# Second-layer chunks of 512 tokens in place of 256, with the second layer's tiles laid over those of attention and the first layer

## The chip, the cores and the metric

The kernel runs on one core of one Trainium2 chip. The time is that of the device for one execution of the program, in microseconds (us). Three runs of the kernel before gave 686.68, 687.62 and 688.28 us; their median, 687.62 us, is what the changed kernel is compared with.

## What is computed

Attention with a sliding window and four sink keys, over 2 sequences of 768 tokens with 8 heads of 64, gives x of 1536 tokens by 512 features. Two feed-forward layers follow, each 512 -> 2048 -> 512. In the second, the hidden values pass through an exponential linear unit. The reference, cut to what matters here:

```python
def _attn_ref(q, k, v, n_sink, window):
    scores = scale * np.matmul(q, k.transpose(0, 1, 3, 2))
    keep = is_sink | in_window
    ...
    return np.matmul(a, v).astype(np.float32)

def _moe_ref(x, w_in, w_out):
    h = x @ w_in
    g = np.where(pos, h, np.where(neg, 0.0, (h + beta) ** 2 / (4.0 * beta)))
    return (g @ w_out).astype(np.float32)

def _moe2_ref(x, w_in, w_out):
    h = x @ w_in
    g = np.where(h > 0.0, h, alpha * (np.exp(np.minimum(h, 0.0)) - 1.0))
    return (g @ w_out).astype(np.float32)
```

## The kernel before

**Tiling.** Tokens lie along the free dimension and features on the partitions. The 1536 tokens are cut into NC = 6 chunks of CT = 256. A product of a layer is made three times over, since every fp32 operand is split into a high and a low part of type fp32r: high x high, high x low, low x high. TensorE holds a 128x128 block of weights and streams one chunk of tokens past it.

**A layer on a chunk.** `layer_chunk` goes over FT = 16 blocks t of the hidden features. `hidden(t)` makes h_t with 12 matmuls (lines 445 to 447: 4 blocks of input features, 3 products each) in one of two PSUM banks `h_ps`. `outward(t)` adds block t to y with 12 matmuls (lines 458 to 460: 4 blocks m of output features, 3 products each). On TensorE the order is hidden(t), outward(t - 2), hidden(t + 1), outward(t - 1) and so on, and a chunk ends with outward(13), outward(14), outward(15). `hidden(t)` waits until VectorE has finished with the bank of h_(t-2) (semaphore `g_ready`); `outward(t)` waits for the low part of g_t (`g_lo_ready`).

**The activation of the second layer.** ScalarE takes relu(-h) into `ramp` (line 589) and exp of its negative into `g_full` (line 591); VectorE makes g = max(e - 1, h) (line 748); ScalarE rounds it to `g_hi` (line 579); VectorE takes the rest, `g_lo` (line 733). g_hi and g_lo are rings of GR = 3 tiles.

**Between chunks.** ScalarE and VectorE split the next chunk's x into `x_hi` (line 573) and `x_lo` (line 728), four blocks k each. ScalarE then waits for the end of outward(15) and copies y out of its two banks, 2 x 512 columns (`write_y`, line 597), since a bank holds two blocks m of 256 tokens. The copies for the last chunk are followed by the last two stores of SyncE's queue (line 336).

**Order of the stages.** Attention of chunk 0 comes first. Attention of chunk c + 1 is then spread over the first layer's chunk c. The last chunk of the first layer has no attention beside it; there the second layer's weights replace the first's, one 128x1024 piece at a time (`split_weights`, lines 563 and 722), and three pieces are left for the second layer's first chunk. Each piece comes by a 512 KB load into one of RAW = 6 raw buffers: two of their own and four lent by tiles of attention. The second layer is the loop `pe.Fori(NC, 2 * NC)` over six chunks.

Every order on an engine is the order in which the code is written; engines meet only at semaphores.

Of the kernel before, what the change touches and what calls it, by code (L numbers as in the profile page):

```python
# [23 lines left out]
F32 = mybir.dt.float32  # L24
# [5 lines left out]
P = 128  # L30
# [5 lines left out]
CPB = SEQ // CT  # L36
QB = CT // P
# [42 lines left out]
def build(nc, q_t, k_t, v_w, v_s, w_in, w_out, ident_d, out, n_sink, window):  # L80
# [8 lines left out]
    with ExitStack() as ctx:  # L89
# [26 lines left out]
        probs_t = sb("probs_t", [P, 2, 512])
        sinks_t, vsink_parts = sb("sinks_t", [P, CT], F32R), sb("vsink_parts", [P, P], F32R)
        masks, mask = sb("masks", [P, 2, QB * MW], BF16), sb("mask", [P, QB * MW], BF16)
# [4 lines left out]
        half = small[:, 4 * QB:4 * QB + 1]  # L123

# [13 lines left out]
        h_ready, y_step = sem("h_ready"), sem("y_step")  # L138
# [11 lines left out]
        def chunk(c):  # L150
            return xy[:, :, bass.ts(c, CT)]
# [40 lines left out]
        def pairs_before(c, p):  # L192
# [14 lines left out]
        place = [i if i < FEW else (i - FEW) % RAW for i in range(NW)] + [i % RAW for i in range(NW)]  # L207
# [49 lines left out]
        def _(sp):  # L257
# [125 lines left out]
        def _(pe):  # L383
# [50 lines left out]
            def hidden(layer, c, t):  # L434
# [5 lines left out]
                o = h_ps[t % 2][:, 0:CT]  # L440
# [9 lines left out]
            def outward(layer, c, t):  # L450


                pe.wait_ge(w_lo_ready, at[layer * NW + 2 * (t // 2) + 1] + 1)
                pe.wait_ge(g_lo_ready, c * FT + (t + 1))
                for m in range(KT):
                    o = y_ps[m // 2][:, (m % 2) * CT:(m % 2 + 1) * CT]
                    cols = slice(m * P, (m + 1) * P)
                    pe.matmul(o, wout_hi[:, t, cols], g_hi[:, t % GR, :], start=(t == 0 and m % 2 == 0), stop=False, skip_group_check=True)  # L458
# [33 lines left out]
            with pe.Fori(NC, 2 * NC) as c:  # L492
                layer_chunk(1, c)
# [3 lines left out]
        def _(act):  # L497
# [67 lines left out]
            def split_x(layer, c, at_chunk, features=range(KT)):  # L565

                for k in features:
                    if layer == 0:
                        act.wait_ge(x_written, c * PAIRS + (k + 1))
                    else:  # L570
                        act.wait_ge(y_written, (at_chunk + 1) * len(y_ps))
# [277 lines left out]
```

## Time and profile before

| what | value |
|---|---|
| median of three runs | 687.62 us (686.68 to 688.28) |
| span of the profiled execution, first to last instruction | 685.2 us |
| its own time, by the span and the about 2.4 us that the median has beyond it | about 687.6 us |
| TensorE matmuls busy | 662.4 us, 97% |
| TensorE weight loads busy | 648.7 us, 95% |
| VectorE busy | 407.8 us, 60% |
| ScalarE busy | 388.3 us, 57% |
| mean granted TensorE clock | 1.000 |

The profile is of one execution. A matmul's recorded duration is modelled and overlaps the next one's, so the pace of TensorE is read from the distance between two starts. PEld is the weight load that goes ahead of each matmul. Busy time is a sum over the whole span; the second layer is the stretch from 403.17 us on.

### The profile page before, as it was taken

Reading aid. Unit: us, or ns where it says so; the run is one execution under the profiler, and the core shown is the slowest. Engines: PE = TensorE matmul, PEld = TensorE weight load, DVE = VectorE, ACT = ScalarE, POOL = GpSimd, SP = SyncE. Lnnn points to the kernel's source line nnn. Section 1 sums busy time; section 2 is a strip of 40 time slices with the busy share of each in tenths; the row PEclk is TensorE's granted clock in tenths of the full one; section 3 lists DMA queues with packets and bytes.
Section 4 is the critical chain, followed back from the end, with each engine's and each line's share of the span. In section 5 each row is a group of like instructions: output and inputs, shape, how many; then the busy total and the mean of one; then the engine's idle time right before and its main releaser. Section 6 shows DMA issues by size and latency. Waiting matters only on the chain.

```text
span 685.2 us, 15326 instructions
## 1 busy us (share of the span) xinstructions
PE 662.4 (97%) x5356; PEld 648.7 (95%) x5356; DVE 407.8 (60%) x1130; ACT 388.3 (57%) x1010; POOL 9.7 (1%) x28
## 2 busy tenths in 40 slices
PE   4889999999999999999999999999999999999997
PEld 3679899999999999999999999999999999999997
DVE  6989976885887588678847864232332322323321
ACT  6877855665656566566655665454454544544443
POOL 3000000000000000000000000000000000000000
PEclk9999999999999999999999999999999999999999
DMA  8468222231332032223125500000000000000000
GB/s 275 170 221 293 67 67 61 76 90 41 89 92 83 23 108 67 65 66 89 43 111 173 182 28 1 2 31 0 0 31 0 31 0 0 31 0 0 31 0 31
DMA packets 27339, 47.39 MB, mean 69 GB/s; under 512 B 2928, under 2 KB 14000, under 8 KB 27312
## 3 DMA queue, kind: packets, MB, share of 16 engines
q1 hardware_dynamic: 27312, 47.03, 22.0%
q8 instruction: 16, 0.26, 0.2%
q14 instruction: 11, 0.09, 0.0%
HBM read 43.88 MB, written 3.15 MB: 69 GB/s over the span
## 4 chain that ended last, share of the span: by engine, by line
PE 87%; DVE 10%; issue 1%; ACT 1%; DMA 0%; ACTq 0%; SPq 0%; DVEq 0%
PE h_ps L445 13%; PE y_ps L458 13%; PE h_ps L447 13%; PE h_ps L446 13%; PE y_ps L460 13%; PE y_ps L459 13%; PE o_ps L424 2%; PE t_ps L403 2%; PE s_ps L391 1%; PE s_ps L392 1%; DVE wout_lo L722 1%; PE o_ps L426 1%; PE o_ps L425 1%; DVE s_ps L676 1%; DVE win_lo L722 1%
## 5 line engine op out<-in xcount | busy, mean ns | idle before, releaser
L445 PE MATMUL h_ps<-x_hi,win_hi 128*128 128x256 f32 x768 | 220.4, 287 | 1.1 <-DVE x_lo L728 0.5
L458 PE MATMUL y_ps<-g_hi,wout_hi 128*128 128x256 f32 x768 | 218.2, 284 | 1.1 <-DVE g_lo L733 1.1
L460 PE MATMUL y_ps<-g_hi,wout_lo 128*128 128x256 f32 x768 | 217.3, 283 | 0.0
L459 PE MATMUL y_ps<-g_lo,wout_hi 128*128 128x256 f32 x768 | 217.3, 283 | 0.0
L447 PE MATMUL h_ps<-x_hi,win_lo 128*128 128x256 f32 x768 | 216.9, 282 | 0.0
L446 PE MATMUL h_ps<-x_lo,win_hi 128*128 128x256 f32 x768 | 216.8, 282 | 0.0
L445 PEld LDWEIGHTS h_ps<-x_hi,win_hi 128*128 128x128 f32 x768 | 146.5, 191 | 3.7 <-DVE g_full L744 1.0
L458 PEld LDWEIGHTS y_ps<-g_hi,wout_hi 128*128 128x128 f32 x768 | 147.3, 192 | 2.7 <-DVE g_lo L733 1.3
L459 PEld LDWEIGHTS y_ps<-g_lo,wout_hi 128*128 128x128 f32 x768 | 147.4, 192 | 0.0
L460 PEld LDWEIGHTS y_ps<-g_hi,wout_lo 128*128 128x128 f32 x768 | 147.3, 192 | 0.0
L446 PEld LDWEIGHTS h_ps<-x_lo,win_hi 128*128 128x128 f32 x768 | 146.8, 191 | 0.0
L447 PEld LDWEIGHTS h_ps<-x_hi,win_lo 128*128 128x128 f32 x768 | 146.7, 191 | 0.0
L748 DVE SCALAR_TENSOR_TENSOR g_full<-g_full,h_ps 128x256 f32<-128x256 f32 x96 | 40.4, 421 | 138.4 <-ACT g_full L591 138.4
L579 ACT CAST g_hi<-g_full 128x256 fp32r<-128x256 f32 x192 | 77.7, 405 | 78.2 <-DVE g_full L748 46.1
L733 DVE TENSOR_TENSOR g_lo<-g_full,g_hi 128x256 fp32r<-128x256 f32 x192 | 81.3, 424 | 67.4 <-ACT g_hi L579 66.7
L589 ACT ACTIVATE ramp<-h_ps 128x256 f32<-128x256 f32 x96 | 36.7, 382 | 88.8 <-PE h_ps L447 88.8
L516 ACT ACTIVATE probs<-s_ps,small 128x260 f32<-128x260 f32 x84 | 39.2, 470 | 22.7 <-DVE small L679 22.6
L586 ACT ACTIVATE ramp<-h_ps,small 128x256 f32<-128x256 f32 x96 | 45.5, 474 | 7.0 <-PE h_ps L447 6.8
L742 DVE SCALAR_TENSOR_TENSOR g_full<-ramp 128x256 f32<-128x256 f32 x96 | 40.4, 420 | 10.2 <-ACT ramp L586 9.8
L744 DVE TENSOR_TENSOR g_full<-g_full,h_ps 128x256 f32<-128x256 f32 x96 | 40.4, 421 | 3.3
L591 ACT ACTIVATE g_full<-ramp 128x256 f32<-128x256 f32 x96 | 40.1, 418 | 3.1
L522 ACT COPY probs_t<-t_ps 128x512 f32<-128x512 f32 x42 | 24.7, 587 | 28.1 <-PE t_ps L403 27.9
(126 smaller groups left out, 704.7 us busy)
## 6 DMA issues: line engine op xcount, KB each, us to landing
ks<-in_k SPq DMA_DIRECT2D x44, 260.0 KB, 2.7
vs<-in_v SPq DMA_DIRECT2D x24, 288.0 KB
qs<-in_q SPq DMA_DIRECT2D x44, 128.0 KB, 2.5
raw<-in_w_in SPq DMA_DIRECT2D x6, 512.0 KB, 4.0
raw<-in_w_out SPq DMA_DIRECT2D x6, 512.0 KB, 4.1
out_y<-xy SPq DMA_DIRECT2D x12, 256.0 KB, 2.3
xy<-in_w_in SPq DMA_DIRECT2D x5, 512.0 KB, 6.3
xy<-in_w_out SPq DMA_DIRECT2D x5, 512.0 KB, 6.7
```

What stands on the lines that cost most here:

```text
L445: pe.matmul(o, win_hi[:, k, f], x_hi[:, k, :], start=(k == 0), stop=False)
L446: pe.matmul(o, win_hi[:, k, f], x_lo[:, k, :], start=False, stop=False)
L447: last = pe.matmul(o, win_lo[:, k, f], x_hi[:, k, :], start=False, stop=(k == KT - 1))
L458: pe.matmul(o, wout_hi[:, t, cols], g_hi[:, t % GR, :], start=(t == 0 and m % 2 == 0), stop=False, skip_group_check=True)
L459: pe.matmul(o, wout_hi[:, t, cols], g_lo[:, t % GR, :], start=False, stop=False, skip_group_check=True)
L460: last = pe.matmul(o, wout_lo[:, t, cols], g_hi[:, t % GR, :], start=False, stop=(t == FT - 1), skip_group_check=True)
L579: nc.scalar.copy(g_hi[:, t % GR, :], g_full[:, t % 2, :]).then_inc(g_hi_ready, 1)
L586: nc.scalar.activation(ramp[:, t % 2, :], h, ACT.Relu, bias=half[:, 0:1], scale=0.5).then_inc(ramp_ready, 1)
L733: nc.vector.tensor_tensor(g_lo[:, t % GR, :], g_full[:, t % 2, :], g_hi[:, t % GR, :].bitcast(F32), ALU.subtract).then_inc(g_lo_ready, 1)
L742: nc.vector.scalar_tensor_tensor(g, r, 1.0, r, ALU.min, ALU.mult).then_inc(bent_ready, 1)
L744: nc.vector.tensor_tensor(g, g, h, ALU.max).then_inc(g_ready, 1)
L748: nc.vector.scalar_tensor_tensor(g, g, -1.0, h, ALU.add, ALU.max).then_inc(g_ready, 1)
```

## The change

The second layer takes chunks of CT1 = 512 tokens, NC1 = 3 of them. Its matmuls stream 512 columns, and its activation, splits and copies are 512 wide. Its tiles (`g1_hi`, `g1_lo`, `ramp1`, `g1_full`, `x1_hi`, `x1_lo`, `raw1`) lie in the SBUF that the tiles of attention and of the first layer held. `ramp1` is one tile where `ramp` had two. The second layer's raw buffers are the two own and three of `raw1`, five where there were six. Each of y's four blocks m has a bank: the two y_ps and the two s_ps, which attention no longer needs. TensorE signals `y_done` as blocks 0 to 2 of a chunk's y are finished, ScalarE copies each when it is there, and each 128x512 block is stored by itself.

```diff
+CT1 = 512
+NC1 = TOK // CT1
...
+        first_layer.close()
+        g1_hi, g1_lo = sb("g1_hi", [P, GR, CT1], F32R), sb("g1_lo", [P, GR, CT1], F32R)
+        ramp1, g1_full = sb("ramp1", [P, 1, CT1]), sb("g1_full", [P, 2, CT1])
+        x1_hi, x1_lo = sb("x1_hi", [P, KT, CT1], F32R), sb("x1_lo", [P, KT, CT1], F32R)
+        raw1 = sb("raw1", [P, 3, KT * GW])
...
+        y1_ps = [*y_ps, *s_ps]
+
+        def layer_tiles(layer):
+
+            if layer == 0:
+                return CT, (x_hi, x_lo), (g_hi, g_lo), ramp, g_full
+            return CT1, (x1_hi, x1_lo), (g1_hi, g1_lo), ramp1, g1_full
+
+        def y_of(layer, m):
+            return y1_ps[m][:, :] if layer else y_ps[m // 2][:, (m % 2) * CT:(m % 2 + 1) * CT]
...
-        lent_late = [ks[:, :, :].rearrange("p s n -> p (s n)")[:, 0:size],
-                     vs[:, :, :, :].rearrange("p s b d -> p (s b d)")[:, 0:size],
-                     probs[:, :, :].rearrange("p j n -> p (j n)")[:, 0:size],
-                     probs_t[:, :, :].rearrange("p h n -> p (h n)")]
+        lent_late = [raw1[:, r, :] for r in range(3)]
+        RAW1 = len(own) + len(lent_late)
...
-        place = [i if i < FEW else (i - FEW) % RAW for i in range(NW)] + [i % RAW for i in range(NW)]
+        place = [i if i < FEW else (i - FEW) % RAW for i in range(NW)] + [i % RAW1 for i in range(NW)]
...
-            with sp.Fori(0, NC) as c:
-                for n in range(len(y_ps)):
-
-                    sp.wait_ge(y_written, (c + NC) * len(y_ps) + (n + 1))
-                    features = slice(2 * n, 2 * n + 2)
-                    sp.dma_start(out[:, features, bass.ts(c, CT)], chunk(c)[:, features, :]).then_inc(stored, 16)
-            sp.wait_ge(stored, 16 * NC * len(y_ps))
+            with sp.Fori(0, NC1) as c:
+                for m in range(KT):
+
+                    sp.wait_ge(y_written, NC * len(y_ps) + (c * KT + (m + 1)))
+                    sp.dma_start(out[:, m, bass.ts(c, CT1)], chunk(c, 1)[:, m, :]).then_inc(stored, 16)
+            sp.wait_ge(stored, 16 * NC1 * KT)
...
-                o = h_ps[t % 2][:, 0:CT]
+                width, (x_hi, x_lo), _, _, _ = layer_tiles(layer)
+                o = h_ps[t % 2][:, 0:width]
...
+                _, _, (g_hi, g_lo), _, _ = layer_tiles(layer)
                 for m in range(KT):
-                    o = y_ps[m // 2][:, (m % 2) * CT:(m % 2 + 1) * CT]
+                    o = y_of(layer, m)
+                    begin = t == 0 and (layer == 1 or m % 2 == 0)
...
+                    if layer == 1 and t == FT - 1 and m < KT - 1:
+                        last.then_inc(y_done, 1)
                 last.then_inc(y_step, 1)
...
-            with pe.Fori(NC, 2 * NC) as c:
+            with pe.Fori(NC, NC + NC1) as c:
                 layer_chunk(1, c)
...
+                for m in range(KT):
+                    if m < KT - 1:
+                        act.wait_ge(y_done, (c - NC) * (KT - 1) + (m + 1))
+                    else:
+                        act.wait_ge(y_step, c * FT + FT)
+                    act.sem_inc(waited_act, 1)
+                    nc.scalar.copy(chunk(at_chunk, 1)[:, m, :], y_of(1, m)).then_inc(y_written, 1)
...
-            with act.Fori(0, NC - 1) as last:
-                between(1, last + NC, last + (NC + 1), last, last + 1)
+            with act.Fori(0, NC1 - 1) as last:
+                between(1, 1, last + NC, last + (NC + 1), last, last + 1)
                 layer_chunk(1, last + (NC + 1))
```

TensorE, the end of a second-layer chunk, outward(15) before: the same instructions as at every t, and y's four blocks in y_ps.

```order
L458 MATMUL y_ps<-g_hi,wout_hi 128x256
L459 MATMUL y_ps<-g_lo,wout_hi 128x256
L460 MATMUL y_ps<-g_hi,wout_lo 128x256
L492 REGISTER_ALU
L492 COMPARE_AND_BRANCH
```

And now; blocks 0 and 1 are in y_ps ahead of these rows, and blocks 2 and 3 in s_ps:

```order
L484 MATMUL s_ps<-g_hi,wout_hi 128x512
L485 MATMUL s_ps<-g_lo,wout_hi 128x512
L486 MATMUL s_ps<-g_hi,wout_lo 128x512
L520 REGISTER_ALU
L520 COMPARE_AND_BRANCH
```

Nothing changes its place; each row is twice as wide, and the branch is taken for three chunks instead of six.

ScalarE, from the last g_hi of the first layer to the second layer's first blocks, before:

```order
L579 CAST g_hi<-g_full 128x256
L573 CAST x_hi<-xy 128x256 x4
L597 COPY xy<-y_ps 128x2x256 x2
L589 ACTIVATE ramp<-h_ps 128x256
L591 ACTIVATE g_full<-ramp 128x256
L579 CAST g_hi<-g_full 128x256
```

And now:

```order
L609 CAST g_hi<-g_full 128x256
L602 CAST x_hi<-xy 128x512 x4
L629 COPY xy<-y_ps 128x2x256 x2
L620 ACTIVATE ramp<-h_ps 128x512
L622 ACTIVATE g_full<-ramp 128x512
L609 CAST g_hi<-g_full 128x512
```

The order is the same; the split of x and the activation are 512 wide. At the very end of ScalarE's program, the last copies before:

```order
L589 ACTIVATE ramp<-h_ps 128x256
L591 ACTIVATE g_full<-ramp 128x256
L648 REGISTER_ALU
L648 COMPARE_AND_BRANCH
L579 CAST g_hi<-g_full 128x256
L597 COPY xy<-y_ps 128x2x256 x2
```

And now:

```order
L620 ACTIVATE ramp<-h_ps 128x512
L622 ACTIVATE g_full<-ramp 128x512
L688 REGISTER_ALU
L688 COMPARE_AND_BRANCH
L609 CAST g_hi<-g_full 128x512
L638 COPY xy<-y_ps 128x512 x2
L638 COPY xy<-s_ps 128x512 x2
```

Two copies of 512 columns behind the last matmul became four, one for each bank, of which three wait for an earlier matmul.

## Rows read from the trace of the kernel before

**Rows 1.** The page: span, busy time by engine.

```profile
span 685.2 us, 15326 instructions
...
PE 662.4 (97%) x5356; PEld 648.7 (95%) x5356; DVE 407.8 (60%) x1130; ACT 388.3 (57%) x1010; POOL 9.7 (1%) x28
```

**Rows 2.** The second layer: us, busy PE, PEld, DVE, ACT, POOL; granted clock, DMA.

```profile
403.17:680.72 277.55, 277.55 (x2306) 276.68 (x2304) 91.75 (x215) 129.78 (x323) 0.00 (x0) 1.00 0.03 10
```

**Rows 3.** Timeline of TensorE around a pause: start, us, instruction.

```profile
401.66 0.36 PE L458 MATMUL y_ps<-g_hi,wout_hi 128*128 128x256 f32 x1
401.86 0.28 PE L459 MATMUL y_ps<-g_lo,wout_hi 128*128 128x256 f32 x1
```

**Rows 4.** Timeline of the weight loads in the same stretch.

```profile
401.63 0.19 PEld L458 LDWEIGHTS y_ps<-g_hi,wout_hi 128*128 128x128 f32 x1 [0.19 <-issue]
401.74 0.19 PEld L459 LDWEIGHTS y_ps<-g_lo,wout_hi 128*128 128x128 f32 x1
401.86 0.19 PEld L460 LDWEIGHTS y_ps<-g_hi,wout_lo 128*128 128x128 f32 x1
```

**Rows 5.** Timeline of TensorE at attention's scores, 260 columns each.

```profile
341.11 0.28 PE L391 MATMUL s_ps<-k_hi,q_parts 128*128 128x260 f32 x1
...
341.58 0.28 PE L445 MATMUL h_ps<-x_hi,win_hi 128*128 128x256 f32 x1
```

**Rows 6.** Timeline of TensorE at attention's values, in plain fp32.

```profile
352.16 0.60 PE L424 MATMUL o_ps<-probs_t,vs 128*128 128x256 f32 x2
352.59 0.38 PE L425 MATMUL o_ps<-probs_t,vs 128*128 128x128 f32 x2
352.81 0.39 PE L426 MATMUL o_ps<-probs_t,vs 128*128 128x128 f32 x2
```

**Rows 7.** Timeline, third block of a second-layer chunk.

```profile
405.93 0.28 PE L447 MATMUL h_ps<-x_hi,win_lo 128*128 128x256 f32 x1
...
406.15 0.39 PE L445 MATMUL h_ps<-x_hi,win_hi 128*128 128x256 f32 x1
...
406.38 0.28 PE L446 MATMUL h_ps<-x_lo,win_hi 128*128 128x256 f32 x1
```

**Rows 8.** Groups of the second layer: busy us, mean ns, idle before.

```profile
L748 DVE SCALAR_TENSOR_TENSOR g_full<-g_full,h_ps 128x256 f32<-128x256 f32 x96 | 40.4, 421 | 138.4 <-ACT g_full L591 138.4
L591 ACT ACTIVATE g_full<-ramp 128x256 f32<-128x256 f32 x96 | 40.1, 418 | 3.1
L579 ACT CAST g_hi<-g_full 128x256 fp32r<-128x256 f32 x96 | 39.0, 406 | 46.1 <-DVE g_full L748 46.1
L589 ACT ACTIVATE ramp<-h_ps 128x256 f32<-128x256 f32 x96 | 36.7, 382 | 88.8 <-PE h_ps L447 88.8
...
L722 DVE TENSOR_TENSOR wout_lo<-vs,wout_hi 128x1024 fp32r<-128x1024 f32 x1 | 1.2, 1225 | 0.5 <-ACT wout_hi L563 0.5
...
L563 ACT CAST wout_hi<-raw 128x1024 fp32r<-128x1024 f32 x1 | 1.0, 1035 | 0.0
```

**Rows 9.** Timelines of loads and casts, and the page's slowest load (us to landing).

```profile
369.59 0.33 SPq L291 DMA_DIRECT2D raw<-in_w_in  x1
...
379.72 1.05 ACT L563 CAST wout_hi<-raw 128x1024 fp32r<-128x1024 f32 x1
...
xy<-in_w_out SPq DMA_DIRECT2D x5, 512.0 KB, 6.7
```

**Rows 10.** Timeline of ScalarE at the start of the second layer.

```profile
400.96 1.32 ACT L573 CAST x_hi<-xy 128x256 fp32r<-128x256 f32 x4
403.45 1.08 ACT L597 COPY xy<-y_ps 128x512 f32<-128x512 f32 x2 [1.16 <-PE y_ps L460]
404.81 0.38 ACT L589 ACTIVATE ramp<-h_ps 128x256 f32<-128x256 f32 x1 [0.28 <-PE h_ps L447]
```

**Rows 11.** Timelines of TensorE and ScalarE at the end.

```profile
680.71 0.28 PE L460 MATMUL y_ps<-g_hi,wout_lo 128*128 128x256 f32 x1
...
681.11 1.07 ACT L597 COPY xy<-y_ps 128x512 f32<-128x512 f32 x2 [2.67 <-PE y_ps L460]
```

More of the change, by code:

```diff
@@ L123, in build, with sb0 @@
         half = small[:, 4 * QB:4 * QB + 1]
+        first_layer = ctx.enter_context(ExitStack())
+        def sb0(name, shape, dt=F32):
+            return first_layer.enter_context(nc.sbuf_tensor(name, shape, dt))
+        x_hi, x_lo = sb0("x_hi", [P, KT, CT], F32R), sb0("x_lo", [P, KT, CT], F32R)
+        g_hi, g_lo = sb0("g_hi", [P, GR, CT], F32R), sb0("g_lo", [P, GR, CT], F32R)
+        ramp, g_full = sb0("ramp", [P, 2, CT]), sb0("g_full", [P, 2, CT])
+        qs, ks = sb0("qs", [P, 2, CT]), sb0("ks", [P, 2, QB * SW])
+        q_parts = sb0("q_parts", [P, CT], F32R)
+        k_hi, k_lo = sb0("k_hi", [P, QB * SW], F32R), sb0("k_lo", [P, QB * SW], F32R)
+        vs = sb0("vs", [P, 2, 3, 3 * HD])
+        vsink = sb0("vsink", [P, 2, P])
+        probs = sb0("probs", [P, QB, 2 * SW])
+        probs_t = sb0("probs_t", [P, 2, 512])
+        sinks_t, vsink_parts = sb0("sinks_t", [P, CT], F32R), sb0("vsink_parts", [P, P], F32R)
+        masks, mask = sb0("masks", [P, 2, QB * MW], BF16), sb0("mask", [P, QB * MW], BF16)
+        first_layer.close()
[3 more added lines that the diff above has]
+        raw1 = sb("raw1", [P, 3, KT * GW])
         h_ps = [ps("h_ps0"), ps("h_ps1")]
@@ L148, in build, with chunk @@
         mask_step, mask_ready = sem("mask_step"), sem("mask_ready")
-        def chunk(c):
-            return xy[:, :, bass.ts(c, CT)]
+        def chunk(c, layer=0):
+            return xy[:, :, bass.ts(c, CT1 if layer else CT)]
+        y1_ps = [*y_ps, *s_ps]
[5 more added lines that the diff above has]
+            return y1_ps[m][:, :] if layer else y_ps[m // 2][:, (m % 2) * CT:(m % 2 + 1) * CT]
         def tiles(parts, first, count, width):
@@ L565, in split_x @@
             def split_x(layer, c, at_chunk, features=range(KT)):
+                _, (x_hi, _), _, _, _ = layer_tiles(layer)
                 for k in features:
@@ L570, in split_x, with part_hi @@
                     else:
-                        act.wait_ge(y_written, (at_chunk + 1) * len(y_ps))
+                        act.wait_ge(y_written, (at_chunk + 1) * (CT1 // CT) * len(y_ps))
                     act.sem_inc(waited_act, 1)
-                    nc.scalar.copy(x_hi[:, k, :], chunk(at_chunk)[:, k, :]).then_inc(x_hi_ready, 1)
-            def part_hi(c, t):
+                    nc.scalar.copy(x_hi[:, k, :], chunk(at_chunk, layer)[:, k, :]).then_inc(x_hi_ready, 1)
+            def part_hi(layer, c, t):
+                _, _, (g_hi, _), _, g_full = layer_tiles(layer)
                 act.wait_ge(g_ready, c * FT + (t + 1))
@@ L582, in activate @@
                 act.wait_ge(h_ready, c * FT + (t + 1))
-                h = h_ps[t % 2][:, 0:CT]
+                width, _, _, ramp, g_full = layer_tiles(layer)
+                h = h_ps[t % 2][:, 0:width]
                 if layer == 0:
@@ L610, in layer_chunk @@
                     if t in PARTS_FIRST:
-                        part_hi(c, t - 1)
+                        part_hi(layer, c, t - 1)
                     if attend is not None:
@@ L722, in split_weights, with split_x, part_lo @@
                 nc.vector.tensor_tensor(lo, src, hi.bitcast(F32), ALU.subtract).then_inc(w_lo_ready, 1)
-            def split_x(c, at_chunk, features=range(KT)):
+            def split_x(layer, c, at_chunk, features=range(KT)):
+                _, (x_hi, x_lo), _, _, _ = layer_tiles(layer)
                 for k in features:
                     dve.wait_ge(x_hi_ready, c * KT + (k + 1))
-                    nc.vector.tensor_tensor(x_lo[:, k, :], chunk(at_chunk)[:, k, :], x_hi[:, k, :].bitcast(F32),
+                    nc.vector.tensor_tensor(x_lo[:, k, :], chunk(at_chunk, layer)[:, k, :], x_hi[:, k, :].bitcast(F32),
                                             ALU.subtract).then_inc(x_lo_ready, 1)
-            def part_lo(c, t):
+            def part_lo(layer, c, t):
+                _, _, (g_hi, g_lo), _, g_full = layer_tiles(layer)
                 dve.wait_ge(g_hi_ready, c * FT + (t + 1))
@@ L748, in activate, with between @@
                     nc.vector.scalar_tensor_tensor(g, g, -1.0, h, ALU.add, ALU.max).then_inc(g_ready, 1)
-            def between(last, c, at_chunk, attend=None):
-                part_lo(last, FT - 1)
-                split_x(c, at_chunk)
+            def between(of_last, layer, last, c, at_chunk, attend=None):
+                part_lo(of_last, last, FT - 1)
+                split_x(layer, c, at_chunk)
                 if attend is not None:
```

76 lines of the change are left out of this document (34 added, 42 removed).

## The prediction

> **What bounds the kernel now.** The page comes first: TensorE's matmuls fill 97% of the span and its weight loads 95%, while VectorE and ScalarE stand at 60% and 57% [rows 1]. Then the second layer alone, which is all that the change touches: 277.55 us from its first matmul to the start of its last, with 2304 weight loads, one for each matmul, and the clock granted at 1.00, its upper level of 2.4 GHz [rows 2]. VectorE works 91.75 us of that and ScalarE 129.78, so TensorE is the limit. The 2303 distances between starts have a mean of 277.54 / 2303 = 0.1205 us. The timeline says what this is made of: 0.12 us from start to start, and one late block in each chunk, where two distances take 406.38 - 405.93 = 0.45 us in place of 0.24 [rows 7]. Six times 0.20 to 0.21 is the 1.2 us by which 277.54 exceeds 2303 x 0.12 = 276.4.
>
> What is to be explained is the 0.12. At 2.4 GHz, 256 columns need 256 / 2.4 = 106.7 ns if one goes in per cycle; 13 ns more pass. Is that a fixed addition to every matmul, a slower stream, or another limit? A pause answers. After it the matmul at 401.66 starts 0.03 us behind its weight load at 401.63. The next weight load begins at 401.74, and the next matmul only at 401.86: 0.20 us after the first [rows 3, 4]. A stream of 256 columns was over by 0.12 at the latest; the second matmul waited for its weights, which take some 0.115 us from the start of their load. The third load begins at 401.86, together with the second matmul [rows 3, 4]. So the steady loop is: a matmul starts, the load for the next one starts with it, and 0.12 us later that load is done and the next matmul starts. The load sets the pace, and the columns hide in it. The four score matmuls fit: with 260 columns each they take 341.58 - 341.11 = 0.47 us, 0.1175 each, no more than 256 columns do [rows 5].
>
> **What 512 columns cost.** No fp32r matmul of 512 columns is in the trace. The nearest row is that of plain fp32. Two L424 matmuls of 256 columns take 352.59 - 352.16 = 0.43 us, and two L425 of 128 columns 352.81 - 352.59 = 0.22 us [rows 6]. That is 0.84 ns per column, two cycles each at 2.4 GHz. So an L424 keeps the array busy for 512 cycles and takes 0.215 us, with a weight load of the same shape wholly inside it. From below the bound is 512 / 2.4 = 213.3 ns; from above, two of today's paces, 240 ns. I take 216 ns, by the row whose array time is the same, with 213.3 to 220 (0.43 is rounded) as its own uncertainty.
>
> The Trainium skill, page "TensorE: Matmul & The Clock Gate", section "Back-to-back issue gap", gives N / 2.4 + 2.5 ns from start to start of matmuls taken alone: 109 ns for 256 columns, 216 for 512. The first differs from this trace (120), whose loads go ahead of each matmul; the second agrees with L424's 215. By it the sum below would be 0.2 us lower.
>
> **The sum.**
> 1. The stream. 2304 matmuls become 1152, with the same products. From the first start to the last: 1151 x 0.216 = 248.6 us in place of 277.5, which had the six late blocks in it. That is **-28.9 us**, of which 1.2 are the late blocks.
> 2. The late block goes. `hidden(2)` waits for g of block 0. From the start of hidden(0)'s last matmul, 403.17 + 11 x 0.12 = 404.49, to the load at 406.15 pass 1.66 us [rows 7, 10], where twelve starts give only 1.44. In this lie relu, exp and VectorE's maximum, 382, 418 and 421 ns for 256 columns [rows 8]. Wider pieces give the slopes: on ScalarE (1035 - 406) / 3 = 210 ns per 256 columns more, on VectorE (1225 - 421) / 3 = 268 [rows 8]. The chain grows by 0.21 + 0.21 + 0.27 and by 0.10 for the longer matmul (two L424 read 0.60, so one reads 0.60 - 0.215 = 0.385, against 0.28 now [rows 6, 7]) to 2.45 us. Twelve starts then give 2.59. It fits by 0.14 us. If it doesn't, three chunks lose some 0.1 to 0.3 us each: up to 0.9 us, kept for the range. Behind that wait stand hidden(2) and outward(0); nothing else waits on them.
> 3. The tail. From the last matmul's start at 680.71 to the span's end at 685.2 are 4.5 us: the copies at 681.11 take 1.07 us, and the last store follows [rows 1, 11]. Three of the four copies now run while TensorE works on later blocks, so one of about 0.59 is left where two took 1.07; the last matmul is 0.10 longer. **-0.4 us.**
> 4. At zero: the split of x. At the first layer's end x_hi starts at 400.96 [rows 10]; 0.40 + 0.21 and 0.42 + 0.27 later x_lo's first block is there, at 402.3, and is wanted at 403.17. The next ones come every 0.6 us and are wanted every 3 x 0.216. Inside the second layer, 37 starts or 8.0 us cover g_15 (2.45), g_hi (0.62) and that 1.3: 3.6 us left. With the cover gone each chunk would pay 1.3.
> 5. At zero: y's copies. At the layer's start they end at 403.45 + 1.08 = 404.5 [rows 10], and hidden(0) now ends at 403.17 + 12 x 0.216 = 405.8. Later only the last 0.6 us copy stands behind outward(15), under 2.6 us of hidden(0). ScalarE's three passes, about 1.9 us a block, and VectorE's two, 1.4, face 24 x 0.216 = 5.2 us, so `ramp1` alone costs nothing either.
> 6. At zero: five raw buffers. SyncE's loads each wait for one split earlier. The seventh piece is cast at 379.72; its load now goes out when the second piece is split, at 369.59, where the eighth's did [rows 9]. That leaves 10.1 us for 512 KB, for which the slowest kind of load needs 6.7 us [rows 9]. The later ones have much the same. Without that cover, every late piece would stop hidden or outward for its lateness.
>
> The profiled execution goes from 685.2 to 685.2 - 28.9 - 0.4 = 655.9 us, and with the 2.4 us between span and median, 687.6 becomes **658.3 us** (-4.3%).
>
> **The rivals.**
> - *Fixed addition.* The 13.3 ns come with every matmul whatever its width: 213.3 + 13.3 = 226.7 ns, 12.3 us more: 670.6. The 0.20 us behind the pause and L424's 0.215 speak against it, but L424 isn't fp32r. 6%.
> - *Slower stream.* An fp32r column costs 120 / 256 = 0.47 ns. Then 512 cost 240 ns, and what is left is the late blocks and the tail: 1151 x 0.240 = 276.2, 685.9 us, next to no change. Against it: 260 columns at 0.1175. For it: that row's four distances are rounded. 3%.
> - *The clock falls (slower).* TensorE streams 106.7 of every 120 ns now and would stream 213 of 216. If that brought the granted clock to 1.2 GHz in part of the second layer, 512 columns would take 427 ns, 0.211 more. 29.3 / 0.211 = 139 matmuls in 1151 at that level, 12%, cancel the gain, and 146 make the kernel slower by 0.2%; half of them give 780 us. Against it: 1.00 through the whole stretch [rows 2]. 3%.
> - *The load stays the pace.* If columns stay hidden in the loop of the weight load at 512 too, 1151 x 0.12 = 138 us, and 548 us in all. L424 at 0.215 with the same load speaks against it, as does the bound of 213.3. 1%. The same section of the Trainium skill states some 131 ns per matmul at 512 columns in a stream with weight loads; that would be 561 us, and no row here shows it.
>
> **How the numbers follow.** The forecast has 87%. Its range takes 213.3 to 220 ns for the matmul (655.2 to 662.9) and up to 0.9 us of step 2 and about 1 us of small waits on top: 655 to 665 us. It leaves out the rivals (13%) and a little of its own case. A measurement of this kernel tells about 0.2% from no change. Faster by more than that are the forecast, the fixed addition, the fourth rival and half of the second: 0.95; within it 0.02; slower, the clock, 0.03.
>
> **What would show it.** Starts of second-layer matmuls 0.216 us apart, with the weight load starting beside the matmul before; 227 or 240 show the first two rivals, a granted clock under 1.00 the third. No distance over 0.22 at hidden(2). Relu, exp and maximum at about 0.59, 0.63 and 0.69 us. TensorE idle in the last first-layer chunk no more than before, without a wait for w_lo. One copy behind the last matmul, and some 4.1 us from its start to the end. The prediction is wrong above all if an fp32r column doesn't go in at one per cycle.

## The result, and the profile after

The changed kernel takes 666.75 us, the median of four runs (665.59 to 667.79), against 687.40 us in the same sessions: a ratio of 0.9702 with a 95% interval of 0.9686 to 0.9717. It is faster by 3.0%. The forecast was 658.3 us and a range of 655 to 665, so the direction was right and the time fell outside the range.

The page of the kernel after, its span and the busy time by engine, which answer to [rows 1]:

```profile
span 665.3 us, 12399 instructions
...
PE 642.4 (97%) x4204; PEld 582.4 (88%) x4204; DVE 390.8 (59%) x1022; ACT 361.6 (54%) x854; POOL 9.4 (1%) x28
```

The second layer now begins at 398.17 us and its last matmul starts at 661.63. This is its stretch, in the columns of [rows 2]:

```profile
398.17:661.64 263.47, 263.47 (x1154) 216.17 (x1152) 75.47 (x109) 102.67 (x168) 0.00 (x0) 1.00 0.02 8
```

1152 weight loads for 2304, at the full clock: 263.46 / 1151 = 228.9 ns from start to start, where 216 was forecast. The part ahead of the second layer, which the change was taken to leave alone, is shorter by 403.17 - 398.17 = 5.0 us. From the last matmul's start to the end 3.7 us pass instead of 4.5. So the span went from 685.2 to 665.3 in three pieces: -5.0, -14.1 and -0.8.

The timelines of TensorE and of its weight loads in the middle of the second layer, after:

```profile
449.91 0.39 PE L470 MATMUL h_ps<-x_lo,win_hi 128*128 128x512 f32 x1
450.14 0.39 PE L471 MATMUL h_ps<-x_hi,win_lo 128*128 128x512 f32 x1
450.37 0.39 PE L484 MATMUL y_ps<-g_hi,wout_hi 128*128 128x512 f32 x1
450.60 0.39 PE L485 MATMUL y_ps<-g_lo,wout_hi 128*128 128x512 f32 x1
```

```profile
449.91 0.19 PEld L471 LDWEIGHTS h_ps<-x_hi,win_lo 128*128 128x128 f32 x1
450.14 0.19 PEld L484 LDWEIGHTS y_ps<-g_hi,wout_hi 128*128 128x128 f32 x1
450.37 0.19 PEld L485 LDWEIGHTS y_ps<-g_lo,wout_hi 128*128 128x128 f32 x1
```

Each load starts with the matmul before the one it is for, as forecast, and a load of 0.19 us lies well inside the 0.23 between starts. Nothing on this timeline waits for another engine; the stream itself takes longer than 213 or 216 ns.

The third block of the second layer's first chunk, after, which answers to [rows 7], and the groups that answer to [rows 8]:

```profile
402.43 0.69 DVE L792 SCALAR_TENSOR_TENSOR g_full<-g_full,h_ps 128x512 f32<-128x512 f32 x1 [3.30 <-ACT g_full L622]
...
403.44 0.39 PE L471 MATMUL h_ps<-x_hi,win_lo 128*128 128x512 f32 x1
403.45 0.19 PEld L469 LDWEIGHTS h_ps<-x_hi,win_hi 128*128 128x128 f32 x1
```

```profile
L792 DVE SCALAR_TENSOR_TENSOR g_full<-g_full,h_ps 128x512 f32<-128x512 f32 x48 | 33.0, 688 | 151.8 <-ACT g_full L622 151.8
L622 ACT ACTIVATE g_full<-ramp 128x512 f32<-128x512 f32 x48 | 30.3, 632 | 1.5
L609 ACT CAST g_hi<-g_full 128x512 fp32r<-128x512 f32 x48 | 29.8, 620 | 34.1 <-DVE g_full L792 34.1
L620 ACT ACTIVATE ramp<-h_ps 128x512 f32<-128x512 f32 x48 | 28.8, 599 | 117.4 <-PE h_ps L471 116.8
```

g of block 0 is ready at 402.43 + 0.69 = 403.12, and hidden(2)'s first load starts at 403.45, beside the matmul before it: the six late blocks of 0.2 us are gone. 599, 632 and 688 ns stand where 0.59, 0.63 and 0.69 us were forecast.

### The profile page after: what moved, and what is told of

Read it like the earlier page. It is cut to its first block, busy times and chain, and to the rows that moved or that the text cites. A ratio compares the mean times of both kernels' runs of the same rounds, so it can differ in the third digit from the quotient of the medians.

```text
span 665.3 us, 12399 instructions
## 1 busy us (share of the span) xinstructions
PE 642.4 (97%) x4204; PEld 582.4 (88%) x4204; DVE 390.8 (59%) x1022; ACT 361.6 (54%) x854; POOL 9.4 (1%) x28
## 4 chain that ended last, share of the span: by engine, by line
PE 85%; DVE 11%; issue 2%; ACT 1%; DMA 1%; SPq 0%; ACTq 0%; DVEq 0%
PE h_ps L469 12%; PE h_ps L471 12%; PE h_ps L470 12%; PE y_ps L484 9%; PE y_ps L486 9%; PE y_ps L485 9%; PE s_ps L486 3%; PE s_ps L485 3%; PE s_ps L484 3%; PE o_ps L447 2%; PE t_ps L426 2%; PE s_ps L414 1%; DVE wout_lo L762 1%; PE s_ps L415 1%; PE o_ps L449 1%
## 5 line engine op out<-in xcount | busy, mean ns | idle before, releaser
L469 PE MATMUL h_ps<-x_hi,win_hi 128*128 128x256 f32 (+1 forms) x576 | 184.5, 320 | 1.3 <-DVE x_lo L769 0.5
L471 PE MATMUL h_ps<-x_hi,win_lo 128*128 128x256 f32 (+1 forms) x576 | 182.7, 317 | 0.0
L470 PE MATMUL h_ps<-x_lo,win_hi 128*128 128x256 f32 (+1 forms) x576 | 182.3, 316 | 0.0
L484 PE MATMUL y_ps<-g_hi,wout_hi 128*128 128x256 f32 (+1 forms) x480 | 145.2, 302 | 1.5 <-DVE g_lo L775 1.3
L486 PE MATMUL y_ps<-g_hi,wout_lo 128*128 128x256 f32 (+1 forms) x480 | 144.9, 302 | 0.0
L485 PE MATMUL y_ps<-g_lo,wout_hi 128*128 128x256 f32 (+1 forms) x480 | 144.6, 301 | 0.0
L469 PEld LDWEIGHTS h_ps<-x_hi,win_hi 128*128 128x128 f32 x576 | 108.1, 188 | 11.1 <-DVE g_full L788 1.1
L775 DVE TENSOR_TENSOR g_lo<-g_full,g_hi 128x256 fp32r<-128x256 f32 (+1 forms) x144 | 73.6, 511 | 53.5 <-ACT g_hi L609 52.9
L609 ACT CAST g_hi<-g_full 128x256 fp32r<-128x256 f32 (+1 forms) x144 | 68.5, 476 | 66.7 <-DVE g_full L792 34.1
L484 PEld LDWEIGHTS y_ps<-g_hi,wout_hi 128*128 128x128 f32 x480 | 90.1, 188 | 7.2 <-issue 1.7
L485 PEld LDWEIGHTS y_ps<-g_lo,wout_hi 128*128 128x128 f32 x480 | 90.1, 188 | 4.2
```

Of the source, the lines that this page charges most:

```text
L469: pe.matmul(o, win_hi[:, k, f], x_hi[:, k, :], start=(k == 0), stop=False)
L470: pe.matmul(o, win_hi[:, k, f], x_lo[:, k, :], start=False, stop=False)
L471: last = pe.matmul(o, win_lo[:, k, f], x_hi[:, k, :], start=False, stop=(k == KT - 1))
L609: nc.scalar.copy(g_hi[:, t % GR, :], g_full[:, t % 2, :]).then_inc(g_hi_ready, 1)
L775: nc.vector.tensor_tensor(g_lo[:, t % GR, :], g_full[:, t % 2, :], g_hi[:, t % GR, :].bitcast(F32), ALU.subtract).then_inc(g_lo_ready, 1)
```

## The experiments

Eleven kernels ran. Four hold streams of matmuls alone; seven are whole kernels. "Place" below is the distance in bytes, modulo 256, from the weights' tiles to the tiles that stream past them. It follows from the order of allocation: for x and g it is 0 in the kernel before and 64 in the changed one, whose `ident` and `small` now lie ahead of x_hi.

**Streams alone.** The core of the first probe, with nothing else running:

```python
for i in range(N):
    f = 0 if same else (i % (weights.shape[1] // P)) * P
    pe.matmul(banks[i % 2][0:cols, 0:moving.shape[1]], weights[:, f:f + cols], moving, start=True, stop=True)
```

> This kernel computes nothing of the reference: it runs streams of 96 matmuls on TensorE, each behind a weight load, while no other engine works, and stores zeros. The moving fp32r tile lies 0, 64, 128, ... 448 bytes further, modulo 512, than the weights; then come widths of 256 and 384, one block of weights used every time, blocks of 64 columns of weights, and bf16. Theory A (a fixed addition of some 13 to 16 ns to every fp32r matmul): 227 to 229 ns at 512 columns wherever the tile lies, 173 to 176 at 384, 120 at 256. Theory B (the weight load and the stream disturb each other by where their tiles lie): the 512-column pace differs by offset, from about 216 to over 229 ns, and the best offset is not 0. Theory C (VectorE's and ScalarE's traffic slows the stream in the kernel): 216 ns at every offset here. Under A the blocks of 64 columns change nothing; if the load disturbs the stream, they bring 512 columns nearer to 216.

Each stretch of its windows holds one stream of 96 matmuls (the counts hold a neighbour or two of the last stream). First 512 columns at places 0, 64, 128 and 192, then 256 and 384 columns at place 0; columns as in [rows 2]:

```profile
38.18:59.96 21.78, 21.78 (x97) 18.02 (x96) 0.00 (x0) 0.00 (x0) 0.00 (x0) 1.00 0.00 0
59.96:81.95 21.99, 21.99 (x97) 18.03 (x96) 0.00 (x0) 0.00 (x0) 0.00 (x0) 1.00 0.00 1
81.95:104.27 22.32, 22.32 (x98) 18.09 (x97) 0.00 (x0) 0.00 (x0) 0.00 (x0) 1.00 0.00 1
104.27:126.66 22.39, 22.39 (x97) 17.95 (x96) 0.00 (x0) 0.00 (x0) 0.00 (x0) 1.00 0.00 1
215.14:226.65 11.51, 11.51 (x98) 11.51 (x96) 0.00 (x0) 0.00 (x0) 0.00 (x0) 1.00 0.00 0
226.65:243.29 16.64, 16.64 (x98) 16.64 (x97) 0.00 (x0) 0.00 (x0) 0.00 (x0) 1.00 0.00 1
```

Divided by 96: 226.9, 229.1, 232.5 and 233.2 ns at 512 columns, 119.9 at 256 and 173.3 at 384. Inside the streams, by single starts, place 0 gives 226.7 and place 64 gives 228.9, which is exactly the changed kernel's pace. So theory C falls: the pace is the same with all other engines idle. Theories A and B both hold in part: at place 0 there is an addition of 13.3 ns at 256, 384 and 512 columns, and the place changes it at 512 (up) and at 256 (down, 117.7 ns at place 64). The same block of weights each time changed nothing (228.9). The bf16 stream ran at 216.

**The first layer's 5 us: place alone.** In the kernel before:

```diff
         xy = sb("xy", [P, KT, TOK])
+        ident = sb("ident", [P, P])
+
+        small = sb("small", [P, 4 * QB + 1])
...
         x_hi, x_lo = sb("x_hi", [P, KT, CT], F32R), sb("x_lo", [P, KT, CT], F32R)
```

> The kernel before with one edit: the tiles ident and small are allocated ahead of x_hi, so that x, g and the tiles behind them lie 576 bytes further (64 modulo 512), as in the changed kernel. Both layers still work on 256 tokens. Theory B: TensorE's pace falls from 119.6 to about 117 ns in the first layer, as in the changed kernel, and falls in the second layer too; 5 us are won in the first part and some 5 to 7 in the second, about 676 us in all. Theories A and C: the pace stays at 120 and the time at 687, and the 5 us that the changed kernel won ahead of its second layer have another cause.

676.39 us, a ratio of 0.9841 (0.9825 to 0.9858), and the second layer starts at 397.25 us, its stretch lasting 272.68 us instead of 277.55:

```profile
397.25:669.93 272.68, 272.68 (x2306) 271.65 (x2304) 91.71 (x215) 130.06 (x323) 0.00 (x0) 1.00 0.03 10
```

Moving the tiles by 576 bytes wins 11 us, with both layers still on 256 tokens. The changed kernel's 5.0 us ahead of its second layer are this; here they are 5.9, and below it shows that the same tiles don't run at one pace in every execution.

**Width alone.** In the changed kernel, `ident` and `small` go from ahead of x_hi to behind the last tile:

```diff
         raw1 = sb("raw1", [P, 3, KT * GW])
+        sb("unused", [P, 328])
+        ident = sb("ident", [P, P])
+
+        small = sb("small", [P, 4 * QB + 1])
```

> The changed kernel with one edit: ident and small lie behind all other tiles, so that x, g, x1 and g1 lie at the same place modulo 512 bytes as the weights, as in the kernel before. The second layer still works on 512 tokens. Theory B: the first part loses its 5 us again, and the 512-column pace is not 229 but higher, toward 240 (twice 120), which would leave the second layer near its old time: 672 to 684 us. Theories A and C: 229 ns in the second layer as in the changed kernel, about 667 us.

669.55 us, 0.9746 (0.9730 to 0.9762). Theory B was right about the first part and wrong about the second: it predicted a slower stream of 512 columns at place 0, and it is the faster one.

```profile
403.01:663.95 260.94, 260.94 (x1154) 216.04 (x1152) 75.43 (x109) 102.65 (x168) 0.00 (x0) 1.00 0.02 8
```

The first part has its old 403.0 us again. The second layer takes 260.94 us, 226.7 ns a matmul. This is the change to 512 tokens without the moved tiles: 687.2 to 669.55, -17.6 us. The two edits together, in the changed kernel, give less than their sum (-17.6 and -10.8), because the gain of place at 256 columns is not had twice, and at 512 columns place 64 costs 2.2 ns.

**What the 13.3 ns are, and where the reading of the pause failed.** The second probe had 48 matmuls per stream and tiles in steps of 32 bytes.

> Streams of 48 matmuls alone, as in the first probe, nothing of the reference computed. Tiles in steps of 32 bytes modulo 256 from the weights, at 512 and 256 columns; fp32r widths 320, 192, 128 and 64; weights moved by 64 bytes with tiles at four places; blocks of 64 weight columns at 256 and 128 columns; plain fp32 at 256; bf16 at 256, 128 and 64; last, groups of six matmuls (512 and 256 columns in turn) with a pause between. Theory A (a fixed 13.3 ns with every fp32r matmul): 146.7 ns at 320 columns, 93.3 at 192, 66.7 at 128; blocks of 64 weights change nothing at 256 columns; behind a pause the second matmul starts some 0.30 us after the first at 512 columns and 0.19 at 256, since the first one's columns wait for its weights. Theory L, that of the prediction (the weight load alone sets the pace at 256 columns): 120 ns at 192, 128 and 64 columns too, about 60 to 90 with 64 weight columns at 256 or 128 columns of stream, and behind a pause 0.22 us at 512. Place: if what counts is the distance from weights to tile, the pattern over the four places turns by 64 bytes with the weights; if the tile's own place counts, it stays.

Its windows, one stream each, in this order: 512, 256, 320, 192 and 128 columns at place 0; 256 columns at place 192 from a second tile of weights; plain fp32 at 256 columns (96 matmuls); bf16 at 256:

```profile
29.56:40.44 10.88, 10.88 (x50) 9.01 (x48) 0.00 (x0) 0.00 (x0) 0.00 (x0) 1.00 0.01 2
118.67:124.42 5.75, 5.75 (x50) 5.74 (x48) 0.00 (x0) 0.00 (x0) 0.00 (x0) 1.00 0.01 3
164.20:171.24 7.04, 7.04 (x50) 7.04 (x49) 0.00 (x0) 0.00 (x0) 0.00 (x0) 1.00 0.01 2
171.24:176.58 5.34, 5.34 (x50) 5.34 (x49) 0.00 (x0) 0.00 (x0) 0.00 (x0) 1.00 0.00 0
176.58:181.91 5.33, 5.33 (x50) 5.33 (x49) 0.00 (x0) 0.00 (x0) 0.00 (x0) 1.00 0.00 0
203.27:208.71 5.44, 5.44 (x49) 5.44 (x48) 0.00 (x0) 0.00 (x0) 0.00 (x0) 1.00 0.00 0
267.64:288.42 20.78, 20.78 (x100) 18.21 (x98) 0.00 (x0) 0.00 (x0) 0.00 (x0) 1.00 0.00 1
288.42:293.66 5.24, 5.24 (x50) 4.70 (x48) 0.00 (x0) 0.00 (x0) 0.00 (x0) 1.00 0.01 3
```

Divided by 48: 226.7, 119.8, 146.7, 111.3 and 111.0 ns; then 113.3; plain fp32 216.5 (215.8 inside the stream) and bf16 109.2. The load does have a pace of its own, 111 to 112 ns, and it shows at 192 and 128 columns (the fourth probe has 111.4 at 224 and 112.0 at 240). It is less than the 120 of 256 columns, so the load alone doesn't set that pace; that it has a part in it, the third probe shows below. Plain fp32 and bf16 add 2.5 ns to their cycles; fp32r adds 13.3 at place 0. Theory A's numbers held at place 0 for 256, 320 and 512 columns, but 192 and 128 columns meet the load's floor first; theory L, the prediction's, wanted 120 there and is out.

Behind a pause (two rows of the same probe, each the first two matmuls of a group, whose time runs from the first start to the second end):

```profile
300.09 0.50 PE L96 MATMUL bank<-at,w 128*128 128x256 f32 x2 [0.71 <-DVE spare L57]
301.79 0.74 PE L96 MATMUL bank<-at,w 128*128 128x512 f32 x2 [0.72 <-DVE spare L57]
```

With 0.28 for one matmul of 256 columns and 0.40 for the second of 512, the second starts 0.22 and 0.34 us after the first. Theory L wanted 0.22 at both widths. What is late is the first stream: its record starts at once, but its columns wait some 0.11 us for its own weights, 0.11 + 0.12 and 0.11 + 0.23.

Place: with a second tile of weights, 64 bytes further, the 512-column pace was 226.7 where the moving tile had moved with them. So the best place goes with the distance and not with the tile's own address. But the distance modulo 256 isn't the whole story. Two windows of 512 columns at place 64, from the first and from the second tile of weights:

```profile
51.64:62.64 11.00, 11.00 (x49) 9.01 (x48) 0.00 (x0) 0.00 (x0) 0.00 (x0) 1.00 0.00 0
225.36:236.56 11.20, 11.20 (x50) 9.08 (x49) 0.00 (x0) 0.00 (x0) 0.00 (x0) 1.00 0.01 1
```

Divided by 48 they are 229.2 and 233.3 ns. At 256 columns place 192 gave 113.3 with the second tile of weights and 117.8 with the first.

**The second layer at place 0, the first at 64.** In the changed kernel:

```diff
         first_layer.close()
+        sb("unused", [P, 48])
         g1_hi, g1_lo = sb("g1_hi", [P, GR, CT1], F32R), sb("g1_lo", [P, GR, CT1], F32R)
```

> The changed kernel with one edit: a gap of 192 bytes ahead of the second layer's tiles, so that they lie at the same place modulo 256 bytes as the weights, while the first layer's tiles stay 64 bytes off. By the first probe (226.7 ns at 0 bytes, 228.9 at 64) the second layer loses 2.2 ns on each of 1151 matmuls, 2.5 us: about 664.2 us. If the place of the tiles matters in no other way than in the probe, the first part stays as in the changed kernel.

663.65 us, 0.9654 (0.9639 to 0.9668); the second layer takes 260.92 us, as with width alone. As expected, 3.1 us under the changed kernel.

**How many weight columns are loaded.**

> Streams of 48 matmuls alone again, nothing of the reference computed, tiles at the same place modulo 256 bytes as the weights; blocks of 128, 96, 64 and 32 weight columns, each at 512 and 256 columns of stream; then sixteen groups of 24 matmuls of 256 columns with a pause between, the tile 64 and 192 bytes off in turn. Theory A1 (13.3 ns belong to the fp32r matmul as such): 226.7 and 120 ns for every number of weight columns. Theory A2 (they are what the weight load of the next matmul takes from the stream that runs beside it, so they shrink with the load): 226.7, 223.3, 220, 216.7 ns at 512 columns and 120, 116.7, 113.3, 110 at 256. The second probe's 60.0 ns at 128 columns with 64 weight columns (53.3 + 6.7) speaks for A2, its 119.0 at 256 for A1, but those tiles lay at other places. Last groups: if the pace depends on place alone, groups with the same tile have the same pace; if it also depends on how a stream began, 113 and 118 both occur.

At place 0, with 96, 64 and 32 weight columns, 512 columns take 230.0, 230.0 and 231.7 ns, and 256 columns 115.9, 113.4 and 113.3. The windows of 256 columns with 128 weight columns, and of 512 and 256 with 64:

```profile
40.86:46.61 5.75, 5.75 (x50) 5.75 (x48) 0.00 (x0) 0.00 (x0) 0.00 (x0) 1.00 0.00 0
...
63.21:74.26 11.05, 11.05 (x50) 6.45 (x49) 0.00 (x0) 0.00 (x0) 0.00 (x0) 1.00 0.00 0
74.26:79.72 5.46, 5.46 (x50) 5.45 (x49) 0.00 (x0) 0.00 (x0) 0.00 (x0) 1.00 0.01 3
```

A2 falls at 512 columns, where a smaller load makes the stream no faster, and A1 at 256, where it does: there half of the 13.3 ns go when the load beside the stream is halved. The last groups of this probe show a second thing: with the same tiles, some groups of 24 settle at 113.3 ns and others at 117.8, already in their first few matmuls, and stay there. Two groups behind a pause, both with the tile at place 192, from the first start to the 24th:

```profile
99.88:102.61 2.73, 2.73 (x24) 2.73 (x24) 0.00 (x0) 0.00 (x0) 0.00 (x0) 1.00 0.02 6
114.93:117.74 2.81, 2.81 (x23) 2.81 (x24) 0.00 (x0) 0.00 (x0) 0.00 (x0) 1.00 0.00 0
```

At place 192 five of eight groups took the faster pace, at place 64 only the one that had no pause ahead of it. The pace also depends on how a stream begins.

**Place at 256 columns, in the kernel before.** Two more orders of allocation, with `masks`, and with `masks` and `ks`, ahead of x_hi and behind `ident` and `small`, which are moved as above:

```diff
+        masks = sb("masks", [P, 2, QB * MW], BF16)
+        ks = sb("ks", [P, 2, QB * SW])
         x_hi, x_lo = sb("x_hi", [P, KT, CT], F32R), sb("x_lo", [P, KT, CT], F32R)
```

> The kernel before, both layers on 256 tokens, with ident, small and masks allocated ahead of x_hi, so that x and g lie 128 bytes modulo 256 from the weights. The probes gave 118.6 ns there at 256 columns, against 120 at 0 and 117.8 at 64: between the kernel before and its version moved by 64 bytes, about 678 to 680 us.

> The same with ks ahead too: x and g lie 192 bytes modulo 256 from the weights. The probes gave 117.8 ns there with one tile of weights and 113.4 with another, so either about 676 us, as moved by 64 bytes, or down to some 656 to 660 us if 113.4 holds through both layers.

Place 128: 683.30 us, 0.9942 (0.9925 to 0.9960), 3 to 5 us more than expected. Place 192: 666.76 us, 0.9708 (0.9691 to 0.9725), between the two cases stated. Its second layer:

```profile
394.48:659.03 264.55, 264.47 (x2306) 263.34 (x2304) 91.80 (x215) 129.98 (x323) 0.00 (x0) 1.00 0.03 10
```

264.55 / 2304 = 114.8 ns a matmul: five of the six chunks run at 113.3, the fifth at 117.8 from its start to its end, and each has its late block. Twenty us of the fourth chunk and twenty of the fifth, the same code on the same tiles:

```profile
550.00:570.00 20.00, 20.00 (x179) 20.00 (x178) 7.36 (x18) 9.34 (x25) 0.00 (x0) 1.00 0.00 0
590.00:610.00 20.00, 20.00 (x172) 20.00 (x172) 5.92 (x14) 8.68 (x22) 0.00 (x0) 1.00 0.00 0
```

The kernel before, on chunks of 256 tokens, thus reaches the changed kernel's time by the order of its allocations alone.

**y's copies.** In the changed kernel, all four copies wait for the end of outward(15), and TensorE no longer signals `y_done`:

```diff
-                    if m < KT - 1:
-                        act.wait_ge(y_done, (c - NC) * (KT - 1) + (m + 1))
-                    else:
-                        act.wait_ge(y_step, c * FT + FT)
+                    act.wait_ge(y_step, c * FT + FT)
```

> The changed kernel with one edit: in the second layer all four copies of y wait for the end of outward(15), none for the matmul that finishes its own block. Behind the last matmul four copies of about 0.5 us each stand where one of 0.6 did, and the last store goes out some 1.5 us later: about 668.2 us. Between chunks the copies end some 2.1 us after outward(15), and relu of block 0 starts at 2.8, so nothing is lost there; if something is, it shows as distances over 0.25 us at hidden(2).

668.06 us, 0.9718 (0.9705 to 0.9731), 1.3 us above the changed kernel. The timelines of ScalarE at the end, of the changed kernel and of this one:

```profile
660.09 1.27 ACT L638 COPY xy<-y_ps 128x512 f32<-128x512 f32 x2 [3.63 <-PE y_ps L486]
661.46 1.27 ACT L638 COPY xy<-s_ps 128x512 f32<-128x512 f32 x2
```

```profile
660.65 1.07 ACT L633 COPY xy<-y_ps 128x512 f32<-128x512 f32 x2 [5.69 <-PE s_ps L486]
661.61 1.09 ACT L633 COPY xy<-s_ps 128x512 f32<-128x512 f32 x2
```

From the last matmul's start (661.63 and 660.14) to the last copy's end pass 1.1 and 2.6 us, and to the end of the span 3.7 and 5.8. The second layer's matmuls keep their 228.9 ns without a late block, so between chunks the copies are hidden either way. The 1.3 us of the times are less than the 2.1 of the tails. This profiled execution has its first part 1.5 us shorter (396.68 against 398.17) with the same tiles. The two paces of 256 columns are the difference: from 356 to 376 us, in the first layer's last chunk, it has 178 weight loads where the changed kernel has 171, that is about 113 ns a matmul for about 117.

**Both layers placed.** The first layer at place 192, by `masks` and `ks` ahead of x_hi, the second at 0, with the second layer's tiles in another order so that each still lies only over what is no longer in use:

```diff
+        sb("unused", [P, 48])
+        x1_lo = sb("x1_lo", [P, KT, CT1], F32R)
+        g1_hi, g1_lo = sb("g1_hi", [P, GR, CT1], F32R), sb("g1_lo", [P, GR, CT1], F32R)
+        g1_full = sb("g1_full", [P, 2, CT1])
+        x1_hi = sb("x1_hi", [P, KT, CT1], F32R)
+        ramp1 = sb("ramp1", [P, 1, CT1])
+        raw1 = sb("raw1", [P, 3, KT * GW])
```

> The changed kernel with its tiles laid out anew and nothing else: masks and ks ahead of x_hi, so that the first layer's x and g lie 192 bytes modulo 256 from the weights, and the second layer's tiles in another order, at 0 bytes. If place is all that these layouts change, the first part is that of the kernel before moved by 192 bytes (its second layer began at 394.5 us, 3.7 us before the changed kernel's), and the second layer runs at 226.7 ns: 2.5 us less. 666.75 - 3.7 - 2.5 = about 660.5 us, under both kernels and under the one with only the second layer placed (663.65). If the gains don't add, it stays at 663 to 664.

661.34 us, 0.9622 (0.9609 to 0.9636): the fastest of all, 5.4 us under the changed kernel.

```profile
395.46:656.36 260.90, 260.90 (x1153) 216.03 (x1152) 75.48 (x109) 102.68 (x169) 0.00 (x0) 1.00 0.02 8
```

**Is the addition counted by 256 columns?**

> Streams of 48 matmuls alone, nothing of the reference computed: fp32r, tile and weights at the same place modulo 256 bytes, 64 weight columns (so that the load sets no pace) at thirteen widths from 512 down to 128, then 128 weight columns at six widths. The probes so far gave, at the best places, 6.7 ns over N / 2.4 at 128 and 256 columns and 13.3 at 320, 384 and 512. Theory Q (6.7 ns for every 256 columns begun): 113.3 ns at 256 with 6.7 more from 257 to 512, so 126.7 at 272 and 133.3 at 288, 106.7 at 240, 100 at 224, 86.7 at 192, 73.3 at 160. Theory F (one fixed 13.3 ns, from which streams of up to 256 columns escape for part of the time): additions that vary between 6.7 and 13.3 with no step at 256.

Neither. With 64 weight columns the additions to N / 2.4 were 6.7 ns at 128, 160, 240 and 256 columns, but 8.5 at 192, 9.9 at 224, 10.6 at 272, 10.0 at 288, 11.1 at 320, 13.3 at 384, 15.7 at 448, 20.0 at 480 and 16.8 at 512. They go up and down with the width, in no clean step. With 128 weight columns 448 had 20.0 and 480 had 16.8. Three of its windows, 512, 256 and 224 columns with 64 weight columns:

```profile
28.59:39.62 11.03, 11.03 (x49) 6.44 (x48) 0.00 (x0) 0.00 (x0) 0.00 (x0) 1.00 0.01 1
87.34:92.79 5.45, 5.45 (x51) 5.45 (x49) 0.00 (x0) 0.00 (x0) 0.00 (x0) 1.00 0.00 0
97.91:102.86 4.95, 4.95 (x51) 4.95 (x50) 0.00 (x0) 0.00 (x0) 0.00 (x0) 1.00 0.00 0
```

## Why the prediction was wrong, step by step

**What bounds the kernel.** That TensorE is the limit was right, and so was the shape of the loop, with each load starting beside the matmul before. "The load sets the pace, and the columns hide in it" was wrong. The load alone would allow 111 to 112 ns; at 256 columns and place 0 the pace is 120, and with half the load beside the same stream 113.3. So the stream, with what the load beside it adds, was the limit, and not the load. The sentence that failed is "the second matmul waited for its weights". The row held the counter-evidence: the first matmul behind the pause reads 0.36 us where the others read 0.28 [rows 3]. Its record began early and its columns late. The second did not wait for its own load; it waited for a stream that had begun 0.1 us behind its record. The probe's pause, 0.34 us at 512 columns, shows it. The fit of 260 columns at 0.1175 [rows 5] was no proof either. It is one group of four: over the whole trace of the kernel before, the median distance behind a k_hi matmul is 122 ns, which is what 260 / 2.4 + 13.3 gives, and 116 to 119 behind a k_lo. And these tiles lie 0 to 48 bytes from q_parts, where x and g lie at 0; in the probes the place moved the pace of 256 columns by several ns.

**Step 1, the stream.** This is the step that failed: 216 ns from plain fp32's row. The term was mis-sized: 1151 x 0.216 = 248.6 us were forecast and 263.46 measured. Plain fp32 does take 215.8 ns for 512 cycles, but fp32r has an addition that plain fp32 and bf16 haven't: 226.7 at place 0. The rival "fixed addition" had named this number and got 6%; its 670.6 us lie 1 us from the 669.55 of width alone. The rest, 2.2 ns a matmul, is place 64. Against the forecast, 10.7 x 1151 = 12.3 us and 2.2 x 1151 = 2.5 us together make the 14.8 by which 263.46 exceeds 248.6. "No fp32r matmul of 512 columns is in the trace" was said, and the range still went only to 220; the trace's own 120 at 256 columns left the addition open, and 240 was written down as the upper bound and not used.

The rule of the Trainium skill that was weighed, N / 2.4 + 2.5 ns (page "TensorE: Matmul & The Clock Gate", section "Back-to-back issue gap"), holds here for bf16 (109.2 at 256 columns, 216 at 512) and for plain fp32 by its cycles, and not for fp32r. The 131 ns of the same section, named beside the fourth rival, was not seen in any stream of 512 columns.

**What the sum left out.** The part ahead of the second layer was taken as untouched. It won 5.0 us, since the diff moves `ident` and `small` ahead of x_hi, and with them every tile of the first layer. The kernel before with only that move (676.39 us, second layer from 397.25) shows it. It is by chance that this made up a third of the shortfall: without it the time would have been further out. In spans, 655.9 was forecast and 665.3 measured, and the 9.4 between them are the 14.8 of step 1 less these 5.0 and 0.4 of step 3. The median lies only 8.4 above its forecast, because it is 1.4 us above this execution's span and not 2.4 as before.

**Step 2, the late block.** Right: gone, worth 1.2 us. The chain was forecast at 2.45 us up to the load. Measured to the end of the maximum it is 403.12 - 400.69 = 2.43 from hidden(0)'s last start (398.17 + 11 x 0.229); before, 0.05 us more passed from there to the load, so 2.48 compare. The slack is some 0.3 us and not 0.14, because the matmuls are slower.

**Step 3, the tail.** The mechanism was right and the size off: -0.75 us (3.7 for 4.46) where -0.4 was forecast. The copies gave what was forecast: the last one ends 1.10 us behind the last matmul's start, where it ended at 1.47. The other 0.38 lie between its end and the end of the span (2.61 for 2.99), which the sum took as unchanged; why that part is shorter is not shown. With all copies at the end the tail is 2.1 longer.

**Steps 4 to 6, at zero.** Right. In the whole second layer no two starts are more than 0.24 us apart, so neither x's split nor y's copies nor `ramp1` is waited for. The first part doesn't lengthen, so the five raw buffers cost nothing; the load for the seventh piece goes out at 365.14 and its cast starts at 375.05, 9.9 us later, where 10.1 were forecast.

**The clock** stayed at 1.00 in the second layer, so the slower rival had no part in it.

**Still open** is what the addition is. The runs exclude other engines' traffic (streams alone show it), a fixed amount for every fp32r matmul (6.7 to 20 ns), an amount proportional to the weight load, and one counted by 256 columns. They show that it depends on the distance between the tile and the weights, though not on that modulo 256 alone (229.2 and 233.3 ns at place 64), at 256 columns on the size of the load, and on how a stream begins. That both are read from SBUF at once, and get in each other's way, would fit that; it was only argued, not shown.

## What to carry to other kernels

When the cost of a wider or narrower instruction decides, measure it by a short stream in a kernel of its own before predicting; a row of another type with the same cycle count is not a measurement. Where a diff moves allocations, take the addresses as part of the change: measure the kernel before with the same moves, or half the effect may be credited to the wrong edit. A matmul record behind a pause starts early; its longer duration says so.

## What the runs showed of the hardware

- The pace of fp32r matmuls depends on where the streamed tile lies relative to the weights. With one tile of weights, 512 columns took 226.7 ns at 0 bytes modulo 256, 228.9 at 64 and 232.5 to 234.2 at the other steps of 32; with a second tile of weights 226.7 at 0 and 233.3 at 64. At 256 columns places 0 and 96 are the slowest, with 120 ns, and 113.3 to 118.6 are had elsewhere. In the kernel before, place alone is worth 20.7 us of 687.45.
- At 256 columns the same tiles run at 113.3 or 117.8 ns, fixed in the first few matmuls of a stream. In the kernel before at place 192 a whole chunk of 384 matmuls keeps the pace that it began with. Two executions with the same first-layer tiles differed by 1.5 us ahead of the second layer.
- Once streams were under way, the granted clock fell only once, in the second probe, in a stream of only 64 fp32r columns a matmul: from its upper level, 2.4 GHz, to its lower, 1.2, and starts 112 ns apart became 213. Before it fell the engine had been loading weights all the time (111 ns a matmul) and streaming columns for less of it, in streams of 192, 128 and 64 columns. It rose again in the next stream, of 512 columns. Two windows of the stream of 64, with the clock in the third column from the end:

```profile
181.91:184.87 2.96, 2.96 (x29) 2.96 (x29) 0.00 (x0) 0.00 (x0) 0.00 (x0) 1.00 0.02 6
184.87:189.40 4.53, 4.53 (x23) 4.53 (x23) 0.00 (x0) 0.00 (x0) 0.00 (x0) 0.50 0.00 0
```

- 2 x 113.3 = 226.7: at its best pace a pair of 256-column matmuls takes exactly what one of 512 takes at its best. What 512 columns bring is that at place 0 they reach it steadily (226.7 in the second layers of three kernels), and half as many waits and loads.
